# A banded attention in front of two expert layers: the second sequence's probabilities are divided on POOL before they are turned, and a query tile's eight heads are weighed in one burst

## The chip, the core and the metric

The kernel runs on one core of a Trainium2 chip. The metric is the device time of one execution in microseconds (us). The engines are TensorE (PE; its weight loads are listed as PEld), VectorE (DVE), ScalarE (ACT), GpSimd (POOL) and SyncE (SP), which here only issues DMAs.

## The reference

```
scores = q @ k^T / sqrt(64)            # batch 2, 8 heads, 768 positions, head width 64
keep   = (key < n_sink) or (0 <= query - key < window)          # n_sink 4, window 128
a      = exp(scores - max) ;  a = a / (sum(a) + 1e-9) ;  x = a @ v
x      = x, as 1536 tokens by 512
h = relu(x @ w_in) ;  x = (h*h) @ w_out                          # layer 1: 512 -> 2048 -> 512
h = x @ w_in2 ;  P, Q polynomials in h ;  out = (P / (Q + 1e-6)) @ w_out2      # layer 2
```

## The kernel before

The 1536 query positions are 12 query tiles of 128 rows, numbered `qt` 0 to 11; tiles 0 to 5 are the first sequence and 6 to 11 the second (`KT` = 6). `i = qt % 6` is a tile's place in its sequence. A unit `u` is one head of one tile (`u = 8*qt + m`, 96 of them), a pair `p` is two neighbouring heads (`PAIRS` = 4 pairs a tile, 48 in all), and a group `g` or `k` is four heads (two a tile, 24 in all). K, Q and V are loaded a group at a time.

For each unit PE makes the scores of the 128 queries against 32 sink columns and two 128-wide key tiles (tile `i = 0` has one, `i < 2` has no sinks); DVE scales, adds the bias and takes the row minimum of the negated scores (L1164); ACT takes the exponential and the row sums (`exp`, L836). Because a key of the two tiles is inside the window in exactly one of them, the later units with sinks (`is_joined`) are folded into one tile of 128 columns first (`join`, L1173) and have 160 columns of probabilities. PE turns the probabilities (`turn_p`, L1503, an identity matmul a tile), ACT copies the turned tiles out of PSUM (`copy_turned`, L814), and for joined units POOL parts them again into the two triangular halves (`halves`, L663, two selects of 128 x 256 a pair). PE then multiplies with V (`weigh_group`, L1546), four heads at a time, each head a 64-column slice of V as the weights, so that `o_ps` receives x already turned: rows are model columns, columns are queries. The multiplications of a group with two key tiles are 8 matmuls, which the profile records as 16, and its sinks 4 more, recorded as 8.

For tiles 3 to 11 the division by the row sums comes last. Since `o_ps` is turned, the inverse sums have to be turned too: DVE inverts the sums (`sums`, L1184), ACT spreads them over 512 columns (`spread`, L868), PE turns these with 4 identity matmuls (`turn_inv`, L1590), ACT copies the result to SBUF (`inv_copy`, L879), and DVE multiplies `o_ps` with it (`divide`, L1220). ACT and DVE then split the quotient into a rounded high part and a low part (`x_high` L884, `x_low` L1225), the operand `xT` of layer 1.

Layer 1 runs over four blocks of three query tiles. In each block are 16 steps `i`; a step is `first1` (12 matmuls, `h_ps`) and `second1` (12 matmuls, `y_ps`), each product made in three passes for precision. Between them `relu` (DVE, L1152), the square and the high part (ACT, L804 and L762) and the low part (DVE, L1111) make the hidden activations; `first1` of step i+1 is issued before `second1` of step i, so this chain has a whole `first1` and `second1` to run beside.

The attention of the next block's tiles is put between these matmuls by `steps` (L262) and `halves_of` (L276). `steps` lists events for blocks 0 to 2: A(n) makes the scores and exponentials of pair n and, for odd n, weighs group (n-3)/2; B(n) turns pair n-1; F(qt) turns a tile's inverse sums. `halves_of` gives every event one of 32 half steps: an even one lies inside `first1`, an odd one in the middle of `second1`. Block 1 carries B(25) to A(37), block 2 B(37) to A(49). M (`divide`), X (`x_high`) and L (`x_low`) hang on A. Every engine walks the same list in order; an engine's `later` part comes at the end of the step. SP issues all loads in one order (L417 to L435): K and Q of group k, then V of group k-1, which waits until groups up to k-3 are weighed (`u_pv`). ACT splits the K and Q of group n/2+2 behind B(n) for odd n (`split_high`, L893).

At the very start POOL makes the mask tiles (`either`, L570), and DVE's first pass over scores waits for them.

Of the kernel before, what the change touches and what calls it, by code (L numbers as in the profile page):

```python
# [14 lines left out]
P = 128  # L15
# [8 lines left out]
GROUP = 4  # L24
# [3 lines left out]
def build(nc, q_cols, k_cols, v_rows, k_pack, q_pack, ks_pack, v_pack, vs_pack, consts_in, w_pack1, w_pack2, out):  # L28
# [28 lines left out]
    JOINED = 4 * H  # L57
    assert DM == 2 * GROUP * D and 2 * D == P and KC == PAIRS and QT == 3 and BLOCKS == 4 and H == 2 * GROUP
# [8 lines left out]
    with ctx:  # L67
# [25 lines left out]
        row_inv = sb("row_inv", [P, H], F32)  # L93

# [51 lines left out]
        rel, sink = sq[:, 0, 0:2 * P], sq[:, 0, 2 * P:3 * P]  # L146
        late, spare = sq[:, 1, 0:2 * P], sq[:, 1, 2 * P:3 * P]

        bpT_of = bpT[:, 0:2 * GROUP * P].rearrange("p (h t n) -> p h t n", h=GROUP, t=2)
# [62 lines left out]

        def score_bank(u):
# [62 lines left out]
        def halves_of(blk):  # L276

            halves = [[] for _ in range(2 * FT)]  # L280
            for e, (kind, n) in enumerate(steps(blk)):
                half = e + (e // 14 if blk else min(e, 1) + e // 6)
                halves[half].append((kind, n))
                if kind == "A" and n % PAIRS == 1:
                    qt = n // PAIRS - 1
                    at_once = half + 2 - half % 2
                    halves[half].append(("M", qt))
                    halves[at_once if qt % QT == QT - 1 else half + 1].append(("X", qt))
                    halves[at_once if qt % QT == QT - 1 else half + 3].append(("L", qt))
            return halves  # L290
# [30 lines left out]
        halves_made = sem("halves_made")  # L321
        u_exp = sem("u_exp")
# [224 lines left out]
        def _(pool):  # L547
# [42 lines left out]
            made(pool.tensor_scalar(masked(0, 0, front), sink[:, 0:SINK_CAP], 1.0, 0.0, ALU.mult, ALU.add))  # L590
# [3 lines left out]
            made(pool.tensor_scalar(masked(1, 0, front), sink[:, 0:SINK_CAP], 1.0, 0.0, ALU.mult, ALU.add))  # L594
# [57 lines left out]
            def banded():  # L652
# [10 lines left out]
                def halves(p):  # L663

                    u = 2 * p
                    i, heads = unit(u)[2], slice(u % GROUP, u % GROUP + 2)
                    pool.wait_ge(pT_by_act, p + 1)
                    pool.wait_ge(u_pv, u // GROUP * GROUP)
                    joined = bprobs[:, u // GROUP % 2, heads, SINK_CAP + P:BAND]
                    pool.affine_select(out=bpT_of[:, heads, i % 2, :], in_=joined, compare_op=ALU.is_ge, fill=0.0,  # L670
                                       base=0, pattern=[[0, 2], [1, P]], channel_multiplier=-1)
                    pool.affine_select(out=bpT_of[:, heads, 1 - i % 2, :], in_=joined, compare_op=ALU.is_ge, fill=0.0,
                                       base=-1, pattern=[[0, 2], [-1, P]], channel_multiplier=1
                                       ).then_inc(halves_made, 1)

# [69 lines left out]
        def _(act):  # L745
# [50 lines left out]
            def banded():  # L796
# [17 lines left out]
                def copy_turned(p):  # L814
# [9 lines left out]
                    else:  # L824
                        act.wait_ge(u_pv, u // GROUP * GROUP)
                        to = bpT_of[:, heads, 0, :] if tiles == 1 else bpT[:, turned_at(u):turned_at(u) + 4 * P]
# [4 lines left out]
                    if with_sinks(u + 1):  # L831
                        act.wait_ge(u_pv, u // GROUP * GROUP)
                        ins = nc.scalar.activation(bpT[:, 2 * GROUP * P:], s_ps[:, 0, 2 * P:3 * P], ACT.Copy)
# [50 lines left out]
                def x_high(qt):  # L884
                    blk, j = divmod(qt, QT)
                    if blk >= 2 and j == 0:
                        act.wait_ge(y_stored, 16 * (blk - 1) + CREDIT)
                    act.wait_ge(o_read, qt + 1)
                    nc.scalar.activation(xT[:, blk % 2, HI, :, j * P:(j + 1) * P],
                                         inv_cols[:, :].rearrange("p (c n) -> p c n", c=KC), ACT.Copy  # L890
# [12 lines left out]
                def step(kind, n):  # L903
                    if kind == "A" and n < P_ALL:
                        exp(2 * n)
                        if 2 * n >= JOINED:
                            exp(2 * n + 1)
                            if with_sinks(2 * n + 1):
                                pack_sinks(n // 2)
                    if kind == "B":  # L910
# [8 lines left out]
                        if n % PAIRS == 0:  # L919
# [143 lines left out]
        def _(dve):  # L1063
# [85 lines left out]
            def banded():  # L1149
# [25 lines left out]

                def pT_part(u):
# [48 lines left out]
                def x_low(qt):  # L1225
                    blk, j = divmod(qt, QT)
                    dve.wait_ge(tile_high, qt + 1)
                    nc.vector.tensor_tensor(xT[:, blk % 2, LO, :, j * P:(j + 1) * P],
                                            inv_cols[:, :].rearrange("p (c n) -> p c n", c=KC),
# [10 lines left out]
                def step(kind, n):  # L1240
# [5 lines left out]
                    if kind == "A" and n % PAIRS == 0:  # L1246
                        sums(n // PAIRS - 1)
                    if kind == "B" and 2 * n - 2 < JOINED:
# [175 lines left out]
        def _(pe):  # L1424
# [77 lines left out]
            def banded():  # L1502
                def turn_p(u):  # L1503
                    i = unit(u)[2]
                    r, mm = u // GROUP % 2, u % GROUP
                    pe.wait_ge(u_exp, u + 1)
# [7 lines left out]
                    if with_sinks(u):  # L1514

                        bank = turn_bank(u) if u < JOINED else s_ps[:, 0, :]
                        qt = u // H
                        pe.wait_ge(sinks_packed, qt // KT * 2 * (KT - 2) + 2 * (i - 2) + u % H // GROUP + 1)
# [27 lines left out]
                def weigh_group(g):  # L1546

                    qt, m, i = unit(GROUP * g)
                    sinks = has_sinks(GROUP * g)
                    if is_joined(GROUP * g):  # L1550
                        pe.wait_ge(halves_made, joined_pairs(2 * g + 1))
                    wait_turned_copies(pe, 2 * g + 1)
                    pe.wait_ge(bv_loaded[g % 4], 16 * (g // 4 + 1))
                    if m == 0:
                        pe.wait_ge(o_read, qt - 1 if qt == QT else qt)
                    tiles = 1 if i == 0 else 2
                    for t in range(tiles):
                        for h in range(m, m + GROUP):
                            rows, at = slice(D * (h % 2), D * (h % 2) + D), turned_at(h) + t * P
                            ins = nc.tensor.matmul(o_ps[rows, h // 2 * P:h // 2 * P + P], bv[:, t, D * h:D * (h + 1)],  # L1560
                                                   bpT[:, at:at + P], start=(h < 2 and t == 0),
                                                   stop=(not sinks and h >= H - 2 and t == tiles - 1),
                                                   skip_group_check=True)
                    if sinks:
                        if i == 2 and m == 0:
                            pe.wait_ge(vs_loaded, 16 * (qt // KT + 1))
                        for h in range(m, m + GROUP):
                            rows = slice(D * (h % 2), D * (h % 2) + D)
                            ins = nc.tensor.matmul(o_ps[rows, h // 2 * P:h // 2 * P + P], bvs[:, D * h:D * (h + 1)],
                                                   bpT[:, 2 * GROUP * P:], start=False, stop=(h >= H - 2),  # L1570
                                                   skip_group_check=True)
                    ins.then_inc(u_pv, GROUP)
# [25 lines left out]
                def step(kind, n):  # L1598
                    if kind == "A":
                        if n < P_ALL:  # L1600
# [7 lines left out]
                            if n % PAIRS == 1:  # L1608
# [3 lines left out]
                        if n % 2:  # L1612
                            weigh_group((n - 3) // 2)
# [198 lines left out]
```

## Time and profile before

| | |
|---|---|
| median of 3 runs | 644.33 us (643.81 to 644.89) |
| the profiled execution | 644.38 us, of which the profile's span is 642.3 us |
| PE busy | 633.8 us (99% of the span) |
| DVE, ACT, POOL busy | 448.5, 389.3, 316.9 us |
| granted TensorE clock | 1.000 of full speed over the whole span |
| the chain that ended last | PE 83%, DVE 11%, ACT 2%, POOL 1% |

Layer 1 with the attention takes the first 371 us, layer 2 the rest. A timeline row gives start and length in us, the engine and line, and how many instructions are merged in it. Matmuls are pipelined and their modelled ends reach into the next row, so the cost of a piece of PE's stream is the distance between starts, not the length of a row.

### The profile page before, as it was taken

How to read it: one execution, taken by the hardware profiler on the slowest of the kernel's cores; microseconds unless marked ns; L12 is line 12 of the kernel's file. 1: busy time of each engine (PE TensorE's matmuls, PEld its weight loads, DVE VectorE, ACT ScalarE, POOL GpSimd, SP SyncE). 2: the span in 40 equal slices, each digit the busy share in tenths (PEclk: the TensorE clock that was granted, in tenths of full speed). 3: DMA queues.
4: the chain of work that ended last, by engine and by line, in shares of the span. 5: the costliest groups of instructions: out<-in, count | busy, mean ns of one | idle time of the engine just before them, and what ended most of it. 6: DMA issues, size and time to landing. Idle time of an engine off the chain costs nothing.

```text
span 642.3 us, 10391 instructions
## 1 busy us (share of the span) xinstructions
PE 633.8 (99%) x3740; PEld 592.1 (92%) x3740; DVE 448.5 (70%) x675; ACT 389.3 (61%) x879; POOL 316.9 (49%) x373
## 2 busy tenths in 40 slices
PE   8999999999999999999999999999999999999997
PEld 6889999999999999999999998888999999999995
DVE  5655656354555545534576799998999988998995
ACT  4755665356545555443222477688777777778774
POOL 6999856000011111110122468777777677776773
PEclk9999999999999999999999999999999999999999
DMA  7786311061111411000434320021000110001001
GB/s 234 245 264 213 112 42 42 1 207 41 42 50 34 138 50 44 10 1 2 119 117 127 98 66 1 1 96 52 1 1 24 76 50 1 0 2 49 1 1 54
DMA packets 28971, 43.49 MB, mean 68 GB/s; under 512 B 4080, under 2 KB 19440, under 8 KB 28400
## 3 DMA queue, kind: packets, MB, share of 16 engines
q1 hardware_dynamic: 28912, 42.74, 20.3%
q8 instruction: 32, 0.52, 0.3%
q14 instruction: 27, 0.22, 0.1%
HBM read 36.44 MB, written 6.29 MB: 67 GB/s over the span
## 4 chain that ended last, share of the span: by engine, by line
PE 83%; DVE 11%; ACT 2%; POOL 1%; issue 1%; DMA 0%; DVEq 0%; ACTq 0%; POOLq 0%; SPq 0%
PE h_ps L1441 24%; PE y_ps L1453 20%; PE y_ps L1744 16%; PE s_ps L1441 8%; PE o_ps L1441 4%; DVE s_ps L1142 4%; PE o_ps L1560 3%; PE s_ps L1494 2%; DVE h_ps L1142 2%; PE s_ps L1513 2%; DVE p_buf L1145 2%; DVE p_buf L1136 1%; PE s_ps L1490 1%; DVE o_ps L1142 1%; PE y_ps L1490 1%
## 5 line engine op out<-in xcount | busy, mean ns | idle before, releaser
L1441 PE MATMUL h_ps<-xT,weights 128*128 128x384 f32 x960 | 189.3, 339 | 0.3 <-DVE sq L1152 0.3
L1441 PEld LDWEIGHTS h_ps<-xT,weights 128*128 128x128 f32 x960 | 167.4, 188 | 4.0 <-issue 2.7
L1453 PE MATMUL y_ps<-hid,weights 128*128 128x384 f32 x768 | 154.1, 341 | 0.0
L1744 PE MATMUL y_ps<-weights,hid 128*128 128x512 f32 x576 | 144.3, 395 | 0.9 <-POOL hid L724 0.4
L1453 PEld LDWEIGHTS y_ps<-hid,weights 128*128 128x128 f32 x768 | 133.8, 188 | 0.9 <-issue 0.9
L1744 PEld LDWEIGHTS y_ps<-weights,hid 128*128 128x128 f32 x576 | 107.1, 188 | 22.9 <-POOL hid L724 2.0
L670 POOL TENSOR_SCALAR_AFFINE_SELECT bpT<-bprobs 128x256 f32<-128x256 f32 x24 | 12.1, 503 | 174.7 <-ACT bprobs L830 124.1
L804 ACT ACTIVATE sq<-sq 128x384 f32<-128x384 f32 x64 | 33.4, 522 | 95.9 <-DVE sq L1152 95.8
L1111 DVE TENSOR_TENSOR hid<-sq,hid 128x384 fp32r<-128x384 f32 x64 | 46.4, 725 | 63.2 <-ACT hid L762 63.1
L724 POOL TENSOR_TENSOR hid<-p_buf,hid 128x384 fp32r<-128x384 f32 x63 | 65.7, 1043 | 42.6 <-ACT hid L1022 42.2
L1142 DVE RECIPROCAL s_ps<-q_buf 128x384 f32<-128x384 f32 x32 | 81.9, 2561 | 3.3
L715 POOL TENSOR_TENSOR q_buf<-h_abs,q_buf 128x384 f32<-128x384 f32 x64 | 65.5, 1023 | 31.1 <-ACT q_buf L780 28.6
L845 ACT ACTIVATE bprobs<-bnegs,neg_max 128x160 f32<-128x160 f32 (+3 forms) x96 | 43.0, 448 | 60.8 <-DVE bnegs L1173 42.1
L1441 PE MATMUL s_ps<-xT,weights 128*128 128x384 f32 x384 | 72.5, 337 | 0.0
L1152 DVE TENSOR_SCALAR sq<-h_ps 128x384 f32<-128x384 f32 x64 | 35.4, 554 | 50.8 <-PE h_ps L1441 50.2
L1441 PEld LDWEIGHTS s_ps<-xT,weights 128*128 128x128 f32 x384 | 68.3, 188 | 2.5
L719 POOL TENSOR_TENSOR p_buf<-p_buf,h_sb 128x384 f32<-128x384 f32 x64 | 66.2, 1034 | 0.0
L600 POOL TENSOR_SCALAR weights<-weights_raw 128x1024 fp32r<-128x1024 f32 x24 | 26.0, 1082 | 61.7 <-DMA weights_raw<-in_w_pack 61.7
L1164 DVE CUSTOM_DVE_ANT_0 bnegs<-s_ps,band_bias 128x288 f32<-128x288 f32 (+2 forms) x81 | 32.0, 425 | 31.1 <-PE s_ps L1494 23.5
L1022 ACT ACTIVATE hid<-p_buf 128x384 fp32r<-128x384 f32 x63 | 33.1, 525 | 28.4 <-DVE p_buf L1145 28.4
L609 POOL TENSOR_TENSOR weights<-weights_raw,weights 128x256 fp32r<-128x256 f32 x64 | 48.8, 795 | 1.0 <-ACT weights L799 0.3
L780 ACT ACTIVATE q_buf<-h_abs,abs_b 128x384 f32<-128x384 f32 x64 | 45.4, 709 | 2.1
(128 smaller groups left out, 885.2 us busy)
## 6 DMA issues: line engine op xcount, KB each, us to landing
weights_raw<-in_w_pack SPq DMA_DIRECT2D x32, 512.0 KB, 4.2
bk_raw<-in_k_pack SPq DMA_DIRECT2D x24, 256.0 KB, 3.5
q_pair<-in_q_pack SPq DMA_DIRECT2D x21, 256.0 KB, 3.4
bv<-in_v_pack SPq DMA_DIRECT2D x24, 128.0 KB, 2.1
y_scratch<-xT SPq DMA_DIRECT2D x2, 1536.0 KB, 6.8
xT<-y_scratch SPq DMA_DIRECT2D x2, 1536.0 KB, 6.6
out_y<-out_stage SPq DMA_DIRECT2D x3, 768.0 KB, 3.5
inv_cols<-in_q_pack SPq DMA_DIRECT2D x3, 256.0 KB, 4.1
```

Of the source, the lines that this page charges most:

```text
L609: ins = pool.tensor_tensor(weights[:, i, LO, c, cols], raw, weights[:, i, HI, c, cols].bitcast(F32), ALU.subtract)
L715: pool.tensor_tensor(q_buf[:, i % RING, :], h_abs[:, i % RING, :], q_buf[:, i % RING, :], ALU.mult).then_inc(qmul_ready, 1)
L719: pool.tensor_tensor(p_buf[:, i % RING, :], p_buf[:, i % RING, :], h_sb[:, i % RING, :], ALU.mult).then_inc(pmul_ready, 1)
L724: pool.tensor_tensor(hid2[:, i % RING, LO, :], p_buf[:, i % RING, :], hid2[:, i % RING, HI, :].bitcast(F32), ALU.subtract).then_inc(hid2_r ...
L780: nc.scalar.activation(q_buf[:, i % RING, :], h_abs[:, i % RING, :], ACT.Identity, scale=abs_b[:, 1:2], bias=abs_b[:, 0:1]).then_inc(lin_r ...
L845: nc.scalar.activation(bprobs[:, u // GROUP % 2, m % GROUP, cols], bnegs[:, neg_slot(u), cols], ACT.Exp, scale=-1.0, bias=neg_max[:, m:m + 1],
L1111: nc.vector.tensor_tensor(hid[:, i % 2, LO, :], sq[:, i % 2, :], hid[:, i % 2, HI, :].bitcast(F32), ALU.subtract).then_inc(hid_ready, 1)
L1142: nc.vector.reciprocal(h_banks[r], q_buf[:, r, :]).then_inc(qinv_ready, 1)
L1152: nc.vector.tensor_scalar(sq[:, i % 2, :], h_ps[:, 0:NT], 0.0, None, ALU.max).then_inc(h_read, 1)
L1441: ins = nc.tensor.matmul(bank, weights[:, i, wp, W_IN, t * P:(t + 1) * P], x, start=(t == 0 and n == 0), stop=(t == KC - 1 and n == 2))
L1453: ins = nc.tensor.matmul(y_ps[:, m, 0:NT], weights[:, i, wp, W_OUT, m * P:(m + 1) * P], hid[:, i % 2, gp, :], start=(i == 0 and n == 0), s ...
L1744: ins = nc.tensor.matmul(y_bank(turn, t), hid2[:, i % RING, gp, t * P:(t + 1) * P], weights[:, i, wp, W_OUT, :], start=(i == 0 and n == 0) ...
```

## The change

`DIVIDED = KT`: everything below holds for tiles 6 to 11. DVE inverts the two sums of a pair in B(n) (two instructions on 128 x 2), POOL multiplies the pair's probabilities in place by them (two instructions, one a unit, each with a per-row scalar), and, for the second pair of a group with sinks, also packs the sinks (which ACT did). PE's turning waits for this instead of for the exponential. The spreading, turning and copying of the inverse sums and the division of `o_ps` are gone, as are the F events; `x_high` and `x_low` read `o_ps`. Both groups of a tile are weighed at one A event, the one that used to weigh the second; the turned probabilities of the two last pairs go to `o_sb` and `inv_cols`, their turned sinks to a free slot of `bnegs`, so eight heads are held at once. Blocks 1 and 2 lay out their 24 events with a gap after every five, where 27 events had one gap after 14. Apart from this, the masks' `sink` and `spare` are 32 columns wide instead of 128, with one instruction more in `either`.

```diff
+    DIVIDED = KT
+        def turned_pair(p):
+            if p // PAIRS >= DIVIDED and p % PAIRS >= 2:
+                return (o_sb, inv_cols)[p % 2][:, :]
+            return bpT[:, p % 2 * 4 * P:(p % 2 + 1) * 4 * P]
+        def weighed_before(u):
+            return u // H * H if u // H >= DIVIDED else u // GROUP * GROUP
 ... steps, halves_of
-                if p % PAIRS == 0:
+                if p % PAIRS == 0 and p // PAIRS - 1 < DIVIDED:
                     found.append(("F", p // PAIRS - 1))
-                half = e + (e // 14 if blk else min(e, 1) + e // 6)
+                half = e + (e // 5 if blk else min(e, 1) + e // 6)
-                    halves[half].append(("M", qt))
+                    if qt < DIVIDED:
+                        halves[half].append(("M", qt))
 ... POOL: masks
-                made(pool.tensor_scalar(spare, of, limits[:, 1:2], 1.0, ALU.is_ge, ALU.mult))
-                made(pool.tensor_tensor(to, spare, sink, ALU.mult))
+                made(pool.tensor_scalar(spare, of[:, 0:SINK_CAP], limits[:, 1:2], 1.0, ALU.is_ge, ALU.mult))
+                made(pool.tensor_tensor(to[:, 0:SINK_CAP], spare, sink, ALU.mult))
+                made(bias(to[:, SINK_CAP:P], of[:, SINK_CAP:P], 1))
 ... POOL: the new division, and its order
+                def divide(p):
+                    pool.wait_ge(pair_inv_made, p - PAIRS * DIVIDED + 1)
+                    for u in (2 * p, 2 * p + 1):
+                        m = u % H
+                        probs = bprobs[:, u // GROUP % 2, u % GROUP, prob_cols(u)]
+                        ins = pool.tensor_scalar(probs, probs, pair_inv[:, m:m + 1], None, ALU.mult)
+                    ins.then_inc(pair_divided, 1)
+                    if with_sinks(2 * p + 1):
+                        pool.wait_ge(pair_divided, p - PAIRS * DIVIDED + 1)
+                        g = p // 2
+                        pool.tensor_scalar(bsinks[:, g % 2, :, :], bprobs[:, g % 2, :, 0:SINK_CAP], 1.0, 0.0, ALU.mult,
+                                           ALU.add).then_inc(sinks_divided, 1)
-                for p in range(JOINED // 2 + 6, P_ALL):
-                    if is_joined(2 * p):
-                        halves(p)
+                halves(JOINED // 2 + 6)
+                for p in range(PAIRS * DIVIDED, P_ALL):
+                    if is_joined(2 * p - 2):
+                        halves(p - 1)
+                    divide(p)
+                halves(P_ALL - 1)
 ... ACT: x_high (x_low on DVE likewise), spread and inv_copy left out
-                    act.wait_ge(o_read, qt + 1)
+                    if qt < DIVIDED:
+                        act.wait_ge(o_read, qt + 1)
+                    else:
+                        act.wait_ge(u_pv, H * (qt + 1))
+                    of = inv_cols if qt < DIVIDED else o_ps
-                        if n % PAIRS == 0:
+                        if n % PAIRS == 0 and n // PAIRS - 1 < DIVIDED:
                             spread(n // PAIRS - 1)
 ... DVE
+                def invert(p):
+                    m, qt = 2 * p % H, 2 * p // H
+                    dve.wait_ge(u_exp, 2 * p + 2)
+                    nc.vector.tensor_scalar(pair_den[:, m:m + 2], row_sum[:, qt % 2, m:m + 2], 1e-9, None, ALU.add
+                                            ).then_inc(pair_den_made, 1)
+                    dve.wait_ge(pair_den_made, p - PAIRS * DIVIDED + 1)
+                    nc.vector.reciprocal(pair_inv[:, m:m + 2], pair_den[:, m:m + 2]).then_inc(pair_inv_made, 1)
+                    if kind == "B" and PAIRS * DIVIDED <= n < P_ALL:
+                        invert(n)
 ... PE
-                    pe.wait_ge(u_exp, u + 1)
+                    if u // H >= DIVIDED:
+                        pe.wait_ge(pair_divided, u // 2 - PAIRS * DIVIDED + 1)
+                    else:
+                        pe.wait_ge(u_exp, u + 1)
-                        if n % 2:
-                            weigh_group((n - 3) // 2)
+                        qt, g = (n - 3) // PAIRS, (n - 3) // 2 % 2
+                        if n % 2 and qt < DIVIDED:
+                            weigh_heads(qt, [g])
+                        elif n % 2 and g == 1:
+                            weigh_heads(qt, [0, 1])
```

`weigh_heads` is `weigh_group` over the heads of one or two groups: the same matmuls on the same operands, key tile by key tile, then all sinks.

## Rows read from the trace of the kernel before

**Rows 1.** Busy time by stretch: us; busy us of PE, PEld, DVE, ACT, POOL; clock; DMA.

```profile
43.00:100.00 57.00, 56.33 (x384) 54.43 (x386) 32.73 (x72) 36.28 (x87) 44.88 (x61) 1.00 0.39 133
130.00:205.00 75.00, 75.00 (x516) 72.64 (x514) 40.54 (x109) 42.39 (x113) 4.20 (x8) 1.00 0.25 80
214.00:293.00 79.00, 79.00 (x565) 76.31 (x565) 40.05 (x102) 40.31 (x112) 11.75 (x24) 1.00 0.15 49
```

**Rows 2.** Chain that ended last, at the end of layer 1: start, us, what.

```profile
366.93 4.24 PE y_ps L1453 x24
...
374.37 2.57 DVE s_ps L1142
```

**Rows 3.** Timeline of PE, plain steps, then a turning of inverse sums.

```profile
120.50 2.24 PE L1441 MATMUL h_ps<-xT,weights 128*128 128x384 f32 x12
122.58 2.28 PE L1453 MATMUL y_ps<-hid,weights 128*128 128x384 f32 x12
124.70 2.24 PE L1441 MATMUL h_ps<-xT,weights 128*128 128x384 f32 x12
...
146.66 1.22 PE L1453 MATMUL y_ps<-hid,weights 128*128 128x384 f32 x6
147.72 0.60 PE L1594 MATMUL s_ps<-ident,o_sb 128*128 128x128 f32 x4
...
149.21 1.21 PE L1441 MATMUL h_ps<-xT,weights 128*128 128x384 f32 x6
```

**Rows 4.** Timeline of PE, three `first1` with scores: weighing 16 records, none, 24.

```profile
176.37 1.20 PE L1441 MATMUL h_ps<-xT,weights 128*128 128x384 f32 x6
...
180.21 1.22 PE L1453 MATMUL y_ps<-hid,weights 128*128 128x384 f32 x6
...
182.54 1.21 PE L1441 MATMUL h_ps<-xT,weights 128*128 128x384 f32 x6
...
185.17 1.22 PE L1453 MATMUL y_ps<-hid,weights 128*128 128x384 f32 x6
...
187.61 1.21 PE L1441 MATMUL h_ps<-xT,weights 128*128 128x384 f32 x6
...
191.89 1.22 PE L1453 MATMUL y_ps<-hid,weights 128*128 128x384 f32 x6
```

**Rows 5.** POOL's `tensor_scalar` with a per-row scalar: ns min/median/max, start, forms.

```profile
L568 POOL TENSOR_SCALAR band_bias<-sq,limits x4: 717/717/1145, 8.1 to 11.4; 128x128 bf16<-128x128 f32 x3, 128x256 bf16<-128x256 f32 x1
```

**Rows 6.** Timeline of PE, POOL and DVE about three turnings of block 2.

```profile
220.56 0.38 PE L1513 MATMUL s_ps<-ident,bprobs 128*128 128x128 f32 x2
...
222.65 0.86 POOL L672 TENSOR_SCALAR_AFFINE_SELECT bpT<-bprobs 128x256 f32<-128x256 f32 x1
...
227.27 0.38 PE L1513 MATMUL s_ps<-ident,bprobs 128*128 128x128 f32 x2
...
228.50 0.41 POOL L672 TENSOR_SCALAR_AFFINE_SELECT bpT<-bprobs 128x256 f32<-128x256 f32 x1
...
234.12 0.80 DVE L1237 TENSOR_TENSOR bq_lo<-q_pair,bq_hi 128x512 fp32r<-128x512 f32 x1
...
234.34 0.85 POOL L672 TENSOR_SCALAR_AFFINE_SELECT bpT<-bprobs 128x256 f32<-128x256 f32 x1
```

**Rows 7.** Timeline of PE: two turnings two half steps apart, no weighing between.

```profile
241.51 0.38 PE L1513 MATMUL s_ps<-ident,bprobs 128*128 128x128 f32 x2
...
246.47 0.38 PE L1513 MATMUL s_ps<-ident,bprobs 128*128 128x128 f32 x2
```

**Rows 8.** Timeline of SP and ACT behind A(29), tile 6's second group.

```profile
152.49 0.62 SPq L430 DMA_DIRECT2D q_pair<-in_q_pack  x1
...
157.62 0.50 ACT L845 ACTIVATE bprobs<-bnegs,neg_max 128x256 f32<-128x256 f32 x1
```

**Rows 9.** DMA issues of block 1: KB each, median us to landing.

```profile
q_pair<-in_q_pack SPq DMA_DIRECT2D x6, 256.0 KB, 3.5
```

**Rows 10.** Timeline at the start: DVE's first pass over scores, its idle time and releaser.

```profile
6.62 0.29 DVE L1164 CUSTOM_DVE_ANT_0 bnegs<-s_ps,band_bias 128x128 f32<-128x128 f32 x1 [1.41 <-POOLq L586]
```

More of the change, by code:

```diff
@@ L589, in _ @@
             pool.sem_inc(masks_made, 1)
[L590 removed]
+            made(pool.tensor_scalar(masked(0, 0, front), sink, 1.0, 0.0, ALU.mult, ALU.add))
             made(bias(masked(0, front, back), own, 1))
@@ L593, in _ @@
             pool.sem_inc(masks_made, 1)
-            made(pool.tensor_scalar(masked(1, 0, front), sink[:, 0:SINK_CAP], 1.0, 0.0, ALU.mult, ALU.add))
+            made(pool.tensor_scalar(masked(1, 0, front), sink, 1.0, 0.0, ALU.mult, ALU.add))
             made(bias(masked(1, front, end), rel, 1))
@@ L1544, in weigh, with weigh_heads @@
                     ins.then_inc(u_pv, 1)
[L1546 to L1555, printed above, removed]
+                def weigh_heads(qt, groups):
+                    i = qt % KT
+                    first, last = H * qt + GROUP * groups[0], H * qt + GROUP * groups[-1] + GROUP - 1
+                    if is_joined(first):
+                        pe.wait_ge(halves_made, joined_pairs(last // 2))
+                    wait_turned_copies(pe, last // 2)
+                    for g in groups:
+                        pe.wait_ge(bv_loaded[(2 * qt + g) % 4], 16 * ((2 * qt + g) // 4 + 1))
+                    if first % H == 0:
+                        if qt <= DIVIDED:
+                            pe.wait_ge(o_read, qt - 1 if qt == QT else qt)
+                        else:
+                            pe.wait_ge(tile_ready, qt)
+                    sinks = has_sinks(first)
                     tiles = 1 if i == 0 else 2
                     for t in range(tiles):
-                        for h in range(m, m + GROUP):
-                            rows, at = slice(D * (h % 2), D * (h % 2) + D), turned_at(h) + t * P
+                        for u in range(first, last + 1):
+                            h = u % H
+                            rows, at = slice(D * (h % 2), D * (h % 2) + D), (u % 2 * 2 + t) * P
                             ins = nc.tensor.matmul(o_ps[rows, h // 2 * P:h // 2 * P + P], bv[:, t, D * h:D * (h + 1)],
-                                                   bpT[:, at:at + P], start=(h < 2 and t == 0),
+                                                   turned_pair(u // 2)[:, at:at + P], start=(h < 2 and t == 0),
                                                    stop=(not sinks and h >= H - 2 and t == tiles - 1),
@@ L1564, in weigh_group @@
                     if sinks:
-                        if i == 2 and m == 0:
+                        if i == 2 and first % H == 0:
                             pe.wait_ge(vs_loaded, 16 * (qt // KT + 1))
-                        for h in range(m, m + GROUP):
+                        for u in range(first, last + 1):
+                            h = u % H
                             rows = slice(D * (h % 2), D * (h % 2) + D)
                             ins = nc.tensor.matmul(o_ps[rows, h // 2 * P:h // 2 * P + P], bvs[:, D * h:D * (h + 1)],
-                                                   bpT[:, 2 * GROUP * P:], start=False, stop=(h >= H - 2),
+                                                   turned_sinks(u), start=False, stop=(h >= H - 2),
                                                    skip_group_check=True)
-                    ins.then_inc(u_pv, GROUP)
+                    ins.then_inc(u_pv, last + 1 - first)
                 def slot(s):
```

48 lines of the change are left out of this document (31 added, 17 removed).

## The prediction

> **What bounds the kernel now.** I read the busy time by stretches first, then the chain that ended last, then PE's timeline in blocks 1 and 2, and last the other engines about single events. In blocks 1 and 2 PE is busy for the whole of both stretches, at full clock, while DVE and ACT have work for about half of the time and POOL for 4 and 12 us [rows 1]. Block 0, where POOL is busy for 45 of 57 us, still leaves PE only 0.7 us idle. So the attention's cost in these blocks is what it puts into PE's stream, and what the other engines do there is free as long as it comes in time. At the end of layer 1 the chain passes from PE's last `second1` to DVE and into DVE's reciprocals [rows 2]. These start a fixed chain after PE ends, so an earlier end of PE moves all of layer 2 forward; I find nothing in layer 2 that waits for a clock of its own.
>
> A busy PE is no measure of cost, so I price by distances between starts. A plain `first1` takes 122.58 - 120.50 = 2.08 us and a plain `second1` 124.70 - 122.58 = 2.12 us [rows 3].
>
> **The change part by part.** *The turning of the inverse sums.* The `second1` that holds it takes 149.21 - 146.66 = 2.55 us, 0.43 more than a plain one [rows 3]. There are six (tiles 6 to 11), and nothing replaces their matmuls: 6 x 0.43 = 2.6 us off PE. The spreading and copying on ACT and the sums and the division on DVE go as well. They lay beside PE and give nothing by themselves, only room.
>
> *One burst for two.* Three `first1` with the same scores in them take 2.63 us without weighing, 3.84 with 16 records and 4.28 with 24 [rows 4]. Eight records thus cost 0.44 us, 24 cost 1.32, and a weighing of 24 costs 1.65: 0.33 us belong to going from the scores to the 64-column products and back. The change keeps every product and makes six bursts fewer: 6 x 0.33 = 2.0 us. From both sides: nothing, if the step from one group to the next costs as much inside a burst, and 2.0 if it costs nothing. I take 2.0, because eight heads in a row are what the 24 records already are, four heads by three tiles, and those run at one pitch of 0.055 us.
>
> *The pair's inverses on DVE.* Two instructions on two columns for each of 24 pairs, with a wait for exponentials made a half step earlier. DVE has 35 to 39 us free in each of these blocks [rows 1], and loses the division and the sums. What is queued behind the wait is the `relu` or the low part, and ACT must finish the same exponentials before it squares. I take 0; without the cover it would be 24 times a few tenths.
>
> *The division on POOL.* This is the new link in front of PE: the turning of pair p in B(p+1) now waits for POOL, and POOL first parts pair p-1, which is turned only in B(p). The trace has no multiplication by a per-row scalar on POOL. The nearest row is a comparison with such a scalar: 0.717 us on 128 columns and 1.145 on 256 [rows 5], that is 0.289 + 0.00334 a column, or 0.82 us on 160. From below, a select of 128 x 256 takes 0.41 us [rows 6], so one on 160 columns may well take under 0.4. I take the upper one for the deadlines, since it is the same instruction form. Then, after a turning of an odd pair (the slow kind: ACT has more to copy), the halves are done at 222.65 + 0.86 - 220.56 = 2.95 us; two divisions and two handovers of 0.05 make 4.70. After a turning of an even pair the halves are done after 228.50 + 0.41 - 227.27 = 1.64 us; two divisions, the packing of sinks (at most the 0.72 of 128 columns) and three handovers make 4.15 [rows 5, 6]. The shortest distance between two turnings, two half steps with scores but no weighing between them, is 246.47 - 241.51 = 4.96 us [rows 7]. By the new list of events, B(38) to B(39) and B(42) to B(43) are this tight behind a slow turning, and six more behind a quick one (from B(33), B(35), B(37), B(43), B(45) and B(47)). The others have an empty half step or the long burst between them, or belong to tiles 6 and 7, where nothing is parted. So POOL is in time everywhere, by 0.3 us at two places and by 0.8 at six.
>
> Here the profile speaks of a danger. The select on 256 columns takes 0.41 us alone and 0.85 beside DVE's subtraction of 0.80 us [rows 6]. If a division meets one at the two tight places, PE waits some 0.15 us each time; I allow 0.2 us in all. The Trainium skill (GPSIMD Engine Reference, Key points) names this: POOL shares its SBUF interfaces with VectorE and contends with DVE instructions that have two SBUF inputs; by that rule, the trace agrees (0.41 against 0.85), and DVE has such instructions in every step. The same page (Engine selection) calls one-input work on POOL roughly line rate, by which POOL would have more than a microsecond to spare at every place; the 3.3 ns a column of the comparison is far from it, and no row shows the multiplication. These two sentences of the page change no term.
>
> *Scores and loads.* The last ones to feel the later weighing are the loads: SP holds V of group k-1 until groups up to k-3 are weighed, and K and Q of group k+1 stand behind it. For an even k-3 in the second sequence that moment is one A event pair later. K and Q of groups 16, 18 and 22 are then issued only behind the long burst of A(29), A(33), A(41), and ACT wants to split them at the end of B(29), B(33), B(41); for group 20 the block's end gives time. At A(29): Q used to be issued there at 152.49 (then for a later group) [rows 8]; with eight records more in the burst it is 152.9, it lands 3.5 us later [rows 9], at 156.4, or 157.4 if the next groups' transfers behind it slow it. Two splits of K and Q and one of sinks follow, up to 1.6 us: ACT is free at 158.0 to 159.0. Its next exponentials began at 157.62 [rows 8] and would begin at 158.06 after the longer burst. So ACT loses 0 to 1 us there. Behind it waits the square for a `second1` that is more than 2 us off, as its `first1` and another half step lie in between. Cost 0, cover some 1 us; without cover up to 1 us each, 3 in all.
>
> *The merged list.* The same A and B events stand in other half steps, with more gaps; a piece costs within 0.04 us the same in either kind of half. The eight-head burst needs both groups' copies, which the second group needed at the same event. At a block's end `x_high` follows the burst without the division: earlier, and behind cover before.
>
> *The masks.* DVE's first pass waits for POOL [rows 10]. Two comparisons shrink from 128 to 32 columns, -0.32 us each, one of 96 is added, +0.61 [rows 5], the product shrinks by something. Between -0.4 and +0.1 us with a handover; I take 0.
>
> The sum: 2.6 + 2.0 - 0.2 = 4.4 us. From the profiled execution's 644.38 us (its span and 2.1 us around it, which stay), 640.0. The median is 0.05 lower, which changes nothing.
>
> **The rivals.** *A: only the inverse turning pays.* The group boundary inside a burst costs what it cost between bursts, because the array is fed from other columns of V and other buffers. For it: I have no row with eight heads. Against: the pitch inside the 24 records is the same over the change from keys to sinks. 644.4 - 2.6 + 0.2 = 642.0.
>
> *B: the loads become the wait.* ACT stands at three splits for K and Q, and PE feels all of it: 3 us lost, 643.0. For it: three transfers more are released at once. Against: the `relu`, square and low-part chain has a `first1` and a `second1` of time.
>
> *C, the other side: POOL is the bound.* Let d be a division on 160 columns. PE waits from d = (4.96 - 2.95 - 0.1)/2 = 0.95 us at two places, and from (4.96 - 1.64 - 0.15 - 0.72)/2 = 1.2 at six. The loss is 4(d - 0.95) + 12(d - 1.2), and it eats the 4.6 us at d = 1.42. If the shared access doubles the 0.82 as it doubled the select, d is 1.65, the loss 8.2 and the time 648.0. For it: DVE has two-input work in each step. Against: only a part of each division can lie beside it, and POOL's price is taken at its upper end.
>
> *D: the change does not do what it says.* PE ends layer 1 earlier and DVE's start into layer 2, or the second weights' loads and POOL's roundings, do not follow: 644.4. Against: all of these wait for PE's progress in block 3.
>
> **How the numbers follow.** Forecast 0.70, A 0.12, B 0.07, C 0.06, D 0.05. The predicted time is 640.0. Its own spread is from 639.3 (no POOL lateness and the masks' 0.4) to 641.0. The range, 639.2 to 642.6, takes in A and leaves out D, C and most of B. A change of 0.2% (1.3 us) is about what the measurement tells from none. Faster by more: forecast, A and half of B, 0.86. Within: D and the rest of B, 0.08. Slower: C, 0.06.
>
> **What would show it.** Right: PE's L1594 has 12 records instead of 36; a `second1` that held it takes 2.12 us or holds one event; an A with eight heads and sinks costs 0.33 + 48 x 0.055 = 3.0 us beyond its scores instead of two times 1.65; PE has no idle time before L1513; blocks 1 and 2 together are 4.4 us shorter and all after them has its old length. Wrong: PE's idle time before L1513 with POOL's division as its releaser (C), ACT's L899 with a DMA as its releaser and PE idle behind it (B), an A burst of 3.3 us (A), or idle PE grown in layer 2 (D).

## The result and the profile after

| | before | after |
|---|---|---|
| median of the runs | 644.33 us (643.81 to 644.89, 5 runs) | 637.14 us (636.71 to 637.71, 5 runs) |
| profiled execution, its span | 644.38 us, 642.3 us | 637.14 us, 635.4 us |

The ratio is 0.9888 [0.9873, 0.9902]: 7.2 us faster. Forecast were 640.0 us and a range of 639.2 to 642.6, so the direction is right and the size is too small by 2.9 us; the time lies below the range.

First the same stretches as in [rows 1]: us; busy us (and records) of PE, PEld, DVE, ACT, POOL; clock; DMA share and GB/s.

```profile
43.00:100.00 57.00, 56.12 (x387) 54.29 (x387) 32.49 (x72) 36.28 (x87) 46.03 (x62) 1.00 0.39 135
130.00:205.00 75.00, 75.00 (x518) 73.61 (x516) 42.33 (x126) 39.76 (x108) 23.31 (x34) 1.00 0.25 75
214.00:293.00 79.00, 78.86 (x565) 77.06 (x564) 40.74 (x115) 34.90 (x98) 28.33 (x52) 1.00 0.16 49
```

POOL has taken over some 17 to 19 us of work in each block, and PE is still busy throughout: nothing that was moved to POOL is felt. As a busy PE says nothing of cost, the difference is read from milestones, the same event in both traces.

| from, to | before | after | after less before |
|---|---|---|---|
| start to the first `first1` (block 0) | 40.08 | 40.49 | +0.4 |
| to a plain `second1` at 118.38 in both | 78.30 | 77.89 | -0.4 |
| to the first plain `first1` behind the last weighing | 174.94 | 170.02 | -4.9 |
| to PE's end in layer 1 | 77.85 | 77.25 | -0.6 |
| to the end of the span | 271.13 | 269.75 | -1.4 |

But for the masks at the very start, the edits should work in the third stretch alone. Of the 6.9 us that the two spans differ by, 2.0 come from the other four rows. Here is PE's timeline of plain steps, answering to [rows 3], with the first plain `first1` behind the last weighing at its end.

```profile
118.38 2.24 PE L1514 MATMUL y_ps<-hid,weights 128*128 128x384 f32 x12
120.46 2.25 PE L1502 MATMUL h_ps<-xT,weights 128*128 128x384 f32 x12
122.55 2.24 PE L1514 MATMUL y_ps<-hid,weights 128*128 128x384 f32 x12
...
288.40 2.25 PE L1502 MATMUL h_ps<-xT,weights 128*128 128x384 f32 x12
```

Read the distances of starts: a plain `second1` takes 120.46 - 118.38 = 2.08 us, where it took 2.12. The `first1` takes 2.09. No instruction of this step was changed, and both run at clock 1.00. The nine matmuls of a step of layer 2 show the same: 503.75 - 501.69 = 2.06 us here, 501.39 - 499.30 = 2.09 before. The two fences are layer 2 of after, then of before.

```profile
501.69 2.22 PE L1817 MATMUL y_ps<-weights,hid 128*128 128x512 f32 x9
503.75 2.27 PE L1502 MATMUL h_ps<-xT,weights 128*128 128x384 f32 x12
```

```profile
499.30 2.25 PE L1744 MATMUL y_ps<-weights,hid 128*128 128x512 f32 x9
501.39 2.27 PE L1441 MATMUL s_ps<-xT,weights 128*128 128x384 f32 x12
```

The burst of eight heads in block 2, from PE's timeline of after: a `first1` with scores only, then one with the scores and all 48 records.

```profile
226.20 1.21 PE L1502 MATMUL h_ps<-xT,weights 128*128 128x384 f32 x6
...
228.83 1.21 PE L1514 MATMUL y_ps<-hid,weights 128*128 128x384 f32 x6
...
231.26 1.21 PE L1502 MATMUL h_ps<-xT,weights 128*128 128x384 f32 x6
...
232.92 0.66 PE L1629 MATMUL o_ps<-bpT,bv 128*64 128x128 f32 x8
233.41 0.39 PE L1629 MATMUL o_ps<-o_sb,bv 128*64 128x128 f32 x4
233.63 0.39 PE L1629 MATMUL o_ps<-inv_cols,bv 128*64 128x128 f32 x4
...
234.72 0.61 PE L1639 MATMUL o_ps<-bpT,bvs 128*64 128x128 f32 x8
235.16 0.61 PE L1639 MATMUL o_ps<-bnegs,bvs 128*64 128x128 f32 x8
...
236.84 1.20 PE L1514 MATMUL y_ps<-hid,weights 128*128 128x384 f32 x6
```

Without weighing 228.83 - 226.20 = 2.63 us, with it 236.84 - 231.26 = 5.58: the burst costs 2.95 us, against 3.0 forecast and two times 1.65 before [rows 4].

The division on POOL, by shapes: count, busy us, mean ns, idle time before and its releaser.

```profile
L706 POOL TENSOR_SCALAR bprobs<-bprobs,pair_inv 128x160 f32<-128x160 f32 x32 | 22.3, 709 | 7.5 <-DVE pair_inv L1232 7.5
L706 POOL TENSOR_SCALAR bprobs<-bprobs,pair_inv 128x256 f32<-128x256 f32 x8 | 7.9, 1000 | 18.0 <-DVE pair_inv L1232 18.0
L706 POOL TENSOR_SCALAR bprobs<-bprobs,pair_inv 128x128 f32<-128x128 f32 x8 | 4.7, 604 | 23.8 <-DVE pair_inv L1232 23.8
```

And the chain that ended last, at the end of layer 1, answering to [rows 2]. It passes from PE to DVE as before; PE's end has moved from 371.17 to 365.65, and DVE's start from 374.37 to 368.86, 5.5 us both times.

```profile
361.48 4.17 PE y_ps L1514 x24
...
368.86 2.57 DVE s_ps L1191
```

### The profile page after: what moved, and what is told of

Read it like the earlier page. It is cut to its first block, busy times and chain, and to the rows that moved or that the text cites. A ratio compares the mean times of both kernels' runs of the same rounds, so it can differ in the third digit from the quotient of the medians.

```text
span 635.4 us, 10375 instructions
## 1 busy us (share of the span) xinstructions
PE 625.5 (98%) x3716; PEld 587.4 (92%) x3716; DVE 447.4 (70%) x705; ACT 380.2 (60%) x859; POOL 354.2 (56%) x431
## 4 chain that ended last, share of the span: by engine, by line
PE 84%; DVE 11%; ACT 2%; issue 1%; POOL 1%; DVEq 0%; ACTq 0%; POOLq 0%
PE h_ps L1502 24%; PE y_ps L1514 20%; PE y_ps L1817 16%; PE s_ps L1502 8%; PE o_ps L1502 4%; DVE s_ps L1191 4%; PE o_ps L1629 3%; PE s_ps L1555 2%; DVE h_ps L1191 2%; PE s_ps L1577 2%; DVE p_buf L1194 2%; DVE p_buf L1185 1%; PE s_ps L1551 1%; DVE o_ps L1191 1%; PE y_ps L1551 1%
## 5 line engine op out<-in xcount | busy, mean ns | idle before, releaser
L1514 PE MATMUL y_ps<-hid,weights 128*128 128x384 f32 x768 | 149.8, 338 | 0.0
L1817 PE MATMUL y_ps<-weights,hid 128*128 128x512 f32 x576 | 142.7, 393 | 1.2 <-POOL hid L765 0.7
L1160 DVE TENSOR_TENSOR hid<-sq,hid 128x384 fp32r<-128x384 f32 x64 | 44.4, 694 | 59.8 <-ACT hid L803 59.8
L706 POOL TENSOR_SCALAR bprobs<-bprobs,pair_inv 128x160 f32<-128x160 f32 (+2 forms) x48 | 35.0, 740 | 49.3 <-DVE pair_inv L1232 49.3
```

The source lines that it names most:

```text
L1160: nc.vector.tensor_tensor(hid[:, i % 2, LO, :], sq[:, i % 2, :], hid[:, i % 2, HI, :].bitcast(F32), ALU.subtract).then_inc(hid_ready, 1)
L1514: ins = nc.tensor.matmul(y_ps[:, m, 0:NT], weights[:, i, wp, W_OUT, m * P:(m + 1) * P], hid[:, i % 2, gp, :], start=(i == 0 and n == 0), s ...
L1817: ins = nc.tensor.matmul(y_bank(turn, t), hid2[:, i % RING, gp, t * P:(t + 1) * P], weights[:, i, wp, W_OUT, :], start=(i == 0 and n == 0) ...
```

## The experiments

Two theories stood. *Places*: the two new tiles of 32 bytes a row, `pair_den` and `pair_inv`, lie ahead of `hid`, so `hid` and what follows stand 64 bytes higher in SBUF, and PE's matmuls on them run at a faster pitch (less time from one to the next); the edits themselves give the 4.4 us forecast. *Edits*: the edits give all of it, because the work of the other engines beside PE's is laid out otherwise. Experiments 1 to 5 decide between them; 6 to 8 test the prediction's own terms. The time beside each result is that of the kernel before, run along with it: it varied from 644.15 to 645.22 us, so single runs are best compared by their traces.

**1. The kernel before with 64 unused bytes ahead of `hid`.**

```
         row_inv = sb("row_inv", [P, H], F32)
+        unused = sb("unused", [P, 16], F32)
```

> The kernel before, with one unused tile of 64 bytes a row in SBUF in front of `hid`, where the change put its two small tiles; no instruction differs. In the changed kernel a plain `second1` takes 2.07 us instead of 2.12 and nine matmuls of layer 2 take 2.06 instead of 2.09, in blocks 0 and 3 too, where no edit reaches. Theory P (place): the 64 bytes by which every later tile moved make this. Then this kernel has the same 2.07 and 2.06, and its time is 644.3 - 64 x 0.045 - 45 x 0.03 = about 640.3 us, at most 641. Rival W (work): PE's matmuls run faster because POOL and the other engines' work lies otherwise. Then it keeps 2.12 and 2.09 and 644.3 us.

Measured: 641.91 us (641.28 to 642.44) beside 645.22, ratio 0.9947 [0.9929, 0.9965]. PE's timeline, layer 1 and layer 2:

```profile
118.96 2.24 PE L1454 MATMUL y_ps<-hid,weights 128*128 128x384 f32 x12
121.03 2.25 PE L1442 MATMUL h_ps<-xT,weights 128*128 128x384 f32 x12
```

The plain `second1` takes 2.07 us, layer 2's nine matmuls 2.06. An unused tile makes the kernel before faster. By milestones behind its start it gains 0.2, 0.5, 0.6 and 1.3 us in the four stretches: 2.7 us, while its start was 0.8 later. The last two are what after gained there (0.6 and 1.4). The whole is less than expected (640.3 us): a plain `second1` gains its 0.04 us, but in the stretches with attention in them the gain is smaller.

**2. The kernel after with the two tiles behind everything else**, so that `hid` stands where it stood before.

```
-        pair_den = sb("pair_den", [P, H], F32)
-        pair_inv = sb("pair_inv", [P, H], F32)
...
+        pair_den = sb("pair_den", [P, H], F32, band)
+        pair_inv = sb("pair_inv", [P, H], F32, band)
```

> The changed kernel with its two small tiles put behind `inv_cols`, so that all tiles of the kernel before lie at their old addresses. Theory P: a `second1` takes 2.12 us again and layer 2's nine matmuls 2.09; the time is 637.1 + 3.3 to 4.2 = 640.4 to 641.3 us, and what is left against 644.3 is what the edits do by themselves. Rival W: 637.1 us as the changed kernel, with 2.07 and 2.06.

Measured: 640.01 us (639.53 to 640.43) beside 645.22, ratio 0.9923 [0.9906, 0.9940]; PE's timeline:

```profile
117.80 2.28 PE L1514 MATMUL y_ps<-hid,weights 128*128 128x384 f32 x12
119.92 2.25 PE L1502 MATMUL h_ps<-xT,weights 128*128 128x384 f32 x12
```

2.12 us again, and 2.09 in layer 2. Against before, the start and the second stretch are 0.3 us shorter each, the third 4.2 shorter, the fourth as long, the last 0.3 longer. So the edits alone give about what was forecast for them. That the median is just the 640.0 forecast is luck: beside its own 645.22 the ratio allows a gain of 3.9 to 6.1 us, where 4.4 were forecast. Behind the start, the two kernels' gains are 2.7 and 4.2 us in the traces, 6.9 together, where after has 7.3: the two effects add to within 0.4 us. The medians can't settle it closer; they give 3.3 and 5.2, 8.5 together against 7.2.

**3. Half of the bytes; twice the bytes.** The same `unused` with 8 and with 32 elements, one run each.

> As e1_before_pad64, with 32 bytes. If it is enough that `hid` does not start at a multiple of 64 bytes (or of 128), the `second1` takes 2.07 us; if 64 is special, 2.12.

> As e1_before_pad64, with 128 bytes. If the place counts only within 128 bytes, it is the kernel before again: `second1` 2.12 us, 644.3 us. If any other place than the old one is better, 2.07 and about 640.5 us. Rival W: 2.12 in all three.

Measured beside 645.22 (644.04 to 646.24): 644.3 us with 32 bytes (`second1` 2.12, nine matmuls 2.10: no gain) and 642.42 with 128 (2.08 and 2.08). 32 bytes are not enough, and the effect has no period of 64 or 128 bytes, since then the kernels moved by 64 or 128 would have been as slow as before.

**4. The 64 bytes behind `hid` and `sq`, ahead of `hid2`.**

> The kernel before, with the 64 unused bytes behind `sq` instead of in front of `hid`: `hid` and `sq` stay, everything behind moves, `hid2` among it. If what counts is the place of the tile that PE itself reads, layer 1 is as before (`second1` 2.12 us, L1 ends as before) and layer 2's nine matmuls take 2.06: 45 x 0.03 = 1.4 us, 643.0 us. If the place of what ACT, DVE and POOL work on counts, layer 1 changes as well.

Measured: 643.27 us in one run beside 644.46. The fence has a plain `second1` and what follows it, then two steps of layer 2.

```profile
118.59 2.28 PE L1454 MATMUL y_ps<-hid,weights 128*128 128x384 f32 x12
120.70 2.24 PE L1442 MATMUL h_ps<-xT,weights 128*128 128x384 f32 x12
...
503.32 2.22 PE L1745 MATMUL y_ps<-weights,hid 128*128 128x512 f32 x9
507.49 2.22 PE L1745 MATMUL y_ps<-weights,hid 128*128 128x512 f32 x9
```

Layer 1 is as before (a `second1` of 2.11), layer 2 has the shorter step (4.17 us from nine matmuls to the next nine, against 4.20 before). So layer 1's step depends on what was moved in experiment 1 and not here (`hid` and `sq`), and layer 2's on what lies behind. PE reads `hid` and `hid2` of these; that it is they, and not `sq` or layer 2's other tiles, which moved with them and which the other engines use, is argued from this and no run separates them.

**5. Other places, in the kernel after.** Unused tiles ahead of `xT` and ahead of `hid`, of so many bytes; the labels give where `xT` and `hid` then stand, modulo 512 (the remainder of the starting byte divided by 512; `hid2` and `hid` have the same). No run shows that 512 is the period; it only names the places. One run each.

> The changed kernel with unused tiles, so that within 512 bytes `xT` begins at 192 (was 128) and `hid`, and with it `hid2`, at 256 (was 64); `weights` stays at 128. So far: `hid` at 0 and 32 gave a `second1` of 2.12 us, at 64 2.07, at 128 2.08; `hid2` there gave 2.09, 2.10, 2.06, 2.08 for nine matmuls of layer 2; `xT` at 128 gives 2.09 for a `first1` and 2.11 in layer 2. If only the 64 bytes behind a 512-byte boundary are bad, `second1` is 2.07 here and `first1` 2.09. If 256 is such a boundary too, 2.12. Time 637.1, or 637.1 + 3.4 at the latter.

> As the one before, with `xT` at 256 and `hid` and `hid2` at 448 within 512 bytes. If 256 is a bad place, `first1` goes from 2.09 to about 2.13 us and layer 2's twelve from 2.11 to 2.15: 128 x 0.04 = 5 us slower, 642 us. If it is only the place within 512, 637.1 us, or less if 64 to 128 bytes from a boundary is what costs the last 0.01.

> The changed kernel with `xT`, `hid` and `hid2` all at 384 within 512 bytes (`weights` at 128). If a tile at the same place as the other operand is best, this is worse than the changed kernel's 4.17 us for a plain `first1` and `second1`; if distance from a 512-byte boundary is what counts, 4.17 or less. 637 to 640 us.

> The changed kernel with `xT` at 64 and `hid` and `hid2` at 192 within 512 bytes. `hid` was best at 64 (2.07 us); if that holds for `xT`, a `first1` goes from 2.09 to 2.07 and layer 2's twelve from 2.11 to 2.09: 128 x 0.02 = 2.5 us, 634.6 us, if 192 is no worse for `hid` than 64. If not, 637 to 640 us.

| `xT`, `hid` modulo 512 | us | plain `first1` + `second1` | `first1` | `second1` | layer 2's nine |
|---|---|---|---|---|---|
| 128, 0 (experiment 2) | 640.01 | 4.20 | 2.08 | 2.12 | 2.09 |
| 128, 64 (after) | 637.14 | 4.17 | 2.09 | 2.07 | 2.06 |
| 192, 256 | 639.72 | 4.19 | 2.08 | 2.10 | 2.09 |
| 256, 448 | 639.53 | 4.19 | 2.10 | 2.08 | 2.09 |
| 384, 384 | 637.53 | 4.16 | 2.08 | 2.08 | 2.08 |
| 64, 192 | 638.11 | 4.17 | 2.10 | 2.08 | 2.10 |

The last three columns are means over the plain steps from 300 to 362 us and over layer 2 from 455 to 620 us, clock 1.00 in both. By and large the time follows the pitch. `weights` stands at 128 throughout. The two rows of 4.19 are slow for different reasons: with `hid` at 256 it is the `second1`, with `xT` at 256 the `first1`. For `second1`, 0 and 32 are the worst places of `hid` and 256 the next; `hid`'s best place, 64, is no good one for `xT` (2.10, where 2.07 was hoped for), and 192 suits `hid` in layer 1 and not `hid2` in layer 2. No two rows but those with distance 0 (the row 384, 384 and experiment 3 with 128 bytes, both 4.16) have the same distance of `hid` from `xT`, so distances aren't tested. What rule lies behind the places stays open. None beats the kernel after.

**6. The eight heads in two bursts again.**

```
-                        if n % 2 and qt < DIVIDED:
+                        if n % 2:
                             weigh_heads(qt, [g])
-                        elif n % 2 and g == 1:
-                            weigh_heads(qt, [0, 1])
```

> The changed kernel with the two groups of a tile weighed at their own A events again, as in the kernel before; all else stays, the places of the tiles too. The prediction priced a burst's coming and going at 0.33 us: then six more bursts make this 2.0 us slower than the changed kernel's 637.1, 639.1 us. If the group boundary costs the same inside a burst (rival A), it is 637.1 us. If the late loads of K and Q, which this edit brings back to their old moments, had cost PE anything (rival B), it is faster than 639.1 by that.

Measured: 640.52 us (639.59 to 641.13) beside 644.15, ratio 0.9945 [0.9925, 0.9965]. The third stretch is 173.03 us, 3.0 longer than after's, where 2.0 were expected. Not all of it is the bursts' price: PE's timeline shows one wait that after doesn't have.

```profile
188.65 1.09 PE L1629 MATMUL o_ps<-bpT,bv 128*64 128x128 f32 x16 [0.97 <-DVE xT L1287]
```

The first burst of a tile writes `o_ps`, which in the kernel after is read by `x_low` itself, without a copy in between. The long burst comes late enough, the early one doesn't. Without this wait six bursts cost 3.01 - 0.97 = 2.04 us, 0.34 each; set against after's turnings, this kernel's fall back by 0.28 to 0.36 us for each of the five tiles without the wait.

**7. The turning of the inverse sums left out of the kernel before.** `x` of the second sequence stays undivided: a copy of `o_ps` stands for the division, and the sums, the spreading, the turning and the copy of the inverses of tiles 6 to 11 go.

```
-                    if kind == "F":
+                    if kind == "F" and n < KT:
...
+                        nc.vector.tensor_copy(inv_cols[:, :], o_ps[:, :]).then_inc(o_read, 1)
```

> The kernel before, with its own places and its own list of events, but for tiles 6 to 11 the inverse sums are neither inverted, spread, turned nor copied, and DVE only copies `o_ps` where it divided: x of the second sequence is left undivided. This is the first term of the prediction alone: 6 x 0.43 = 2.6 us off PE, 644.3 - 2.6 = 641.7 us, with the second1 of 2.55 us at 2.12. If the ACT and DVE work that goes as well had cost PE time, it is below 641.5; if the four matmuls were hidden by a wait that stays, 644.3.

Measured: 641.4 us (640.76 to 642.06) beside 644.46, ratio 0.9955 [0.9939, 0.9972]. The `second1` that held the turning, on PE's timeline:

```profile
146.49 2.28 PE L1457 MATMUL y_ps<-hid,weights 128*128 128x384 f32 x12
148.61 1.21 PE L1445 MATMUL h_ps<-xT,weights 128*128 128x384 f32 x6
```

148.61 - 146.49 = 2.12, a plain one, and the third stretch is 172.29, 2.65 us shorter: six times 0.44. The work that went from ACT and DVE with it gave nothing more.

**8. Each division done twice** (first into a scratch tile), to see what a slower POOL would do.

```
...
+                        pool.tensor_scalar(scratch[:, 0:cols.stop - cols.start], probs, pair_inv[:, m:m + 1], None,
+                                           ALU.mult).then_inc(scratched, 1)
```

> The changed kernel, with every division on POOL made twice, once into a tile that nobody reads. It doubles the link in front of PE's turning. A division on 160 columns takes 0.71 us in the changed kernel. By the prediction's deadlines (4.96 us between two close turnings) the two slow places then need 2.95 + 0.1 + 2.84 = 5.9 us and the six quick ones 1.64 + 2.84 + 0.55 = 5.0, so PE stands some 1 us at each of two and a little at six: 2 to 2.5 us, 639.1 to 639.6. If POOL was a half step further ahead than I worked out, PE does not stand and it is 637.1 us.

Measured: 640.44 us, one run, later than the 639.1 to 639.6 expected. PE's waits from 120 to 300 us, and the timeline of POOL ahead of the longest:

```profile
PE s_ps L1584 <- POOL bprobs L713: 2.1, 3, 1.0
PE h_ps L1509 <- DVE sq L1208: 0.3, 1, 0.3
```

```profile
163.64 1.06 POOL L711 TENSOR_SCALAR scratch<-bprobs,pair_inv 128x256 f32<-128x256 f32 x1
164.68 0.92 POOL L713 TENSOR_SCALAR bprobs<-bprobs,pair_inv 128x256 f32<-128x256 f32 x1
```

The mechanism of rival C is real: PE stands before the turning and POOL releases it. Two of the waits are at places that C named, B(37) to B(38) with 0.27 us and B(38) to B(39) with 0.86. The longest is not: 0.98 us at 165.75, in tile 7, behind divisions of 256 columns, which take 0.92 to 1.06 us each and four of them for a pair; POOL had stood 5.5 us for DVE's inverses ahead of them, so there it started late and wasn't behind with other work. And B(42) to B(43), called as tight as B(38) to B(39), shows no wait. The third stretch grew by 3.7 us. The idle time shown is not all that a wait costs: set against after's, this kernel's turnings fall back by 1.14, 0.40 and 1.13 us at these three places, 2.7 in all. The `relu` ahead of one `first1` costs 0.2 more than in after, and the other 0.8 come in small steps without a wait that the profile names. Undoubled, the division causes none of these waits.

## Why the prediction was too small

*The turning of the inverse sums, -2.6.* Right. L1664 has 12 records, and experiment 7 measures 2.65 us for it alone.

*One burst for two, -2.0.* Right. The burst costs 2.95 us as forecast, and experiment 6 finds 0.34 us for each burst more. Rival A, that the boundary between groups costs as much inside a burst, would have made it 3.3. The records show the turned matrices of four pairs, from three buffers, at one pitch.

*POOL's lateness, 0.2 us of loss.* It was 0: PE has no wait on POOL between 120 and 300 us. At B(38) to B(39), one of the two tight places, the chain can be followed in POOL's timeline of after, behind the turning at 217.80:

```profile
219.44 0.49 POOL L694 TENSOR_SCALAR_AFFINE_SELECT bpT<-bprobs 128x256 f32<-128x256 f32 x1 [2.35 <-ACT bpT L878]
219.89 0.85 POOL L696 TENSOR_SCALAR_AFFINE_SELECT bpT<-bprobs 128x256 f32<-128x256 f32 x1
221.07 1.34 POOL L706 TENSOR_SCALAR bprobs<-bprobs,pair_inv 128x160 f32<-128x160 f32 x2 [0.32 <-DVE pair_inv L1232]
```

The halves are done 2.94 us behind the turning (forecast 2.95), the divisions at 4.61 (forecast 4.70), and the next turning comes at 222.86, 5.06 behind. The division is cheaper than its bound, here 1.34 us for two against 2 x 0.82, but 0.32 us of waiting for DVE's inverse, which the sum did not have, uses up part of that. Rival C needed 0.95 us for a division. The danger that the prediction spoke of is real but falls elsewhere: where two divisions begin beside DVE's subtraction, they take 1.76 and 1.77 us instead of 1.34. That comes twice among the pairs of 160 columns, and both times the next turning is 2.6 us or more behind their end. DVE's and POOL's timelines of after:

```profile
232.43 0.80 DVE L1296 TENSOR_TENSOR bq_lo<-q_pair,bq_hi 128x512 fp32r<-128x512 f32 x1
232.67 1.76 POOL L706 TENSOR_SCALAR bprobs<-bprobs,pair_inv 128x160 f32<-128x160 f32 x2
```

*The inverses on DVE, 0.* Nearly: one place lost 0.3 us. DVE's and PE's timelines of after:

```profile
256.34 2.24 PE L1514 MATMUL y_ps<-hid,weights 128*128 128x384 f32 x12
...
257.55 0.37 DVE L1229 TENSOR_SCALAR pair_den<-row_sum 128x2 f32<-128x2 f32 x1
257.95 0.17 DVE L1232 RECIPROCAL pair_inv<-pair_den 128x2 f32<-128x2 f32 x1
258.03 0.54 DVE L1201 TENSOR_SCALAR sq<-h_ps 128x384 f32<-128x384 f32 x1
...
258.72 0.58 PE L1502 MATMUL h_ps<-xT,weights 128*128 128x384 f32 x2
```

Two tiny instructions, 0.48 us with their handovers, stand ahead of the `relu`; the next `first1` starts 2.38 us behind the `second1` instead of 2.08.

*Loads, 0.* Right: ACT does wait for K, at the place named, and PE doesn't feel it. ACT's timeline of after:

```profile
155.44 0.63 ACT L948 ACTIVATE bkT<-bk_raw 128x512 fp32r<-128x512 f32 x1 [0.95 <-DMA bk_raw<-in_k_pack]
155.98 0.61 ACT L950 ACTIVATE bq_hi<-q_pair 128x512 fp32r<-128x512 f32 x1
156.50 0.40 ACT L984 ACTIVATE bkT<-bk_raw 128x256 fp32r<-128x256 f32 x1
156.81 0.49 ACT L890 ACTIVATE bprobs<-bnegs,neg_max 128x256 f32<-128x256 f32 x1
```

K has landed by 155.44, a microsecond before the 156.4 that the forecast gave Q, and the exponentials begin at 156.81 instead of 158.06. Rival B was unfounded.

*The masks, 0.* Not settled. DVE's first pass begins at 6.55 us, 0.07 earlier, and waits for PE's scores there and no longer for POOL, so this wait can't give more. The first `first1` of block 0 falls between 39.8 and 40.9 us over the kernels run, with the new masks both early (39.77 in experiment 2) and late (40.49 in after), so this variation hides it.

*The sum.* Edits: -2.65 - 2.04 and the `relu`'s +0.3 are -4.4; experiment 2 measures -4.2 in the third stretch. That this is the -4.4 of the forecast is in part luck: the 0.2 us that it allowed for POOL didn't come, and 0.3 that it didn't have came on DVE. **The step that failed is the last one**, "all after them has its old length", and with it the tacit term of 0 for the two new tiles. The prediction priced instructions and waits, and left out that a tile of 32 bytes, twice, moves every later tile. By experiment 1 that is worth 2.7 us behind the start, by the difference of after and experiment 2 it is 3.1 (2.9 by their medians), which is about the 2.9 us by which the forecast was too small. Of experiment 1's 2.7 some 1.3 us are in layer 2 (64 times nine matmuls) and 0.6 in block 3; the rest is in the stretches with attention in them, where it is less than 0.04 us for each `second1`. Why these places are faster for PE stays open. The profile before could not have given the size. It did show that there was something to ask: `first1` and `second1` are both twelve matmuls of 384 columns, and one took 0.04 us longer than the other [rows 3].

## What to carry to other kernels

When a change adds, drops or resizes a tile, compare the starting address of every later tile that the bound engine reads (the engine that sets the time, PE here), and where they differ run the kernel before with an unused tile of the same size: it splits the gain of the edit from that of the places. Compare in the trace the distance of starts of steps that the change does not touch; a difference there is no part of the edit. And put the small instructions of a new chain behind the ones on which the bound engine waits: 0.5 us on two columns cost PE more than 17 us on another engine.

## What the runs showed of the hardware

- In this kernel PE's pitch depended on where tiles stand in SBUF. Twelve matmuls of 384 columns took 2.12 us with `hid` at 157696 bytes of each row (0 modulo 512) and with 32 bytes more, and 2.07 to 2.08 with 64 or 128 more; nine of 512 columns in layer 2, whose `hid2` moves alike, took 2.09 to 2.10 and 2.06 to 2.08. The granted clock was 1.00 in all stretches compared. In this kernel that is half a per cent of the time.
- POOL's multiplication by a per-row scalar took 0.60, 0.71 and 1.00 us on 128, 160 and 256 columns in the mean. The means hold some that stood beside a DVE instruction with two SBUF inputs; alone it took 0.60, 0.68 and 0.92 us, that is 0.28 us and 2.5 ns a column. That is nearer to the comparison's price [rows 5] than to the lone select's of 0.41 [rows 6].
- Going from 128x128 products to 64-column ones and back cost 0.31 to 0.34 us, whatever the number of records between: 2.95 - 48 x 0.055 = 0.31 with 48, 0.33 with 16 and 24 [rows 4], and 0.34 for each burst more in experiment 6.
